# In each expert slot, y's squares and y's scaled copy move ahead of both halves of the next second weight's conversion

## The chip, the cores and the metric

The kernel runs on one core of one Trainium2 chip. The metric is the device time of one execution in microseconds (us), lower is better. In a program on one core that is the core's own time. The engines are named as in the profile: PE is TensorE, DVE is VectorE, ACT is ScalarE, POOL is GpSimd, SP is SyncE. ACTq and SPq stand for the queues from which ACT and SP issue transfers.

## What is computed

The reference is three layers in a row. The change touches only the second.

```python
# 1. attention with a state per head: for every step t (S = 768), B = 4, H = 8, D = 48
y[:, :, t] = einsum('bhd,bhde->bhe', q[:, :, t], state)
state = state + bt * einsum('bhd,bhe->bhde', kt, vt - einsum('bhde,bhd->bhe', state, kt))
# 2. mixture of 8 experts, one for each token: x [3072, 384], w1 [8, 384, 1024], w2 [8, 1024, 384]
expert_idx = argmax(logits, axis=1)
for e in range(E):
    h = maximum(x[mask] @ w1[e], 0.0)
    out[mask] = gate_w[mask, None] * (h @ w2[e])
# 3. dense: w_in [384, 2048], w_out [2048, 384]
h = maximum(x @ w_in, 0.0)
return h * h @ w_out
```

## The kernel before

The program has three stages, one for each layer, each with a stream of instructions for every engine; semaphores set all order between engines. The order within an engine is the order in which its function is written, and an instruction that waits holds back everything written behind it on that engine.

The second stage, `experts`, is a loop over NS = 31 slots. A slot is a tile of 128 tokens that all go to one expert. Its work, for slot j:

- PE: `up(j)` is x @ w1 in two halves of 24 matmul passes each (L1356). Then `turn_x(j + 1)` transposes the next tile's x (L1345). Then `down(j)` is h @ w2, 24 matmuls of 384 columns (L1367): each of the 8 blocks of h takes three, since h and w2 are both held as a high and a low part. `down(j)` waits for both parts of the first half of h (`s_ht[0]`), for the low part of the first half of w2 (`s_w2_lo`), and for the y of the slot before (`s_ys`). After 12 of its matmuls it waits again, for the second halves. `down` is followed by `up(j + 1)` with nothing between.
- ACT: `high_h(j, 0)` and `high_h(j, 1)` write the high part of h (L1406), each when PE's half of `up(j)` is done. `take_xt(j + 1)` copies the transposed x (L1393). Then come `high_w2(j + 1, 0)` and `high_w2(j + 1, 1)`, which convert the two halves of the next slot's second weight to its high part (L1402), and `square_y(j)` (L1422), which takes the sum of the squares of y. At the end ACT waits for the scaled y and issues its store (L1448).
- DVE: `low_h(j, 0)` and `low_h(j, 1)` write the low part of h (L1473). `low_w2(j + 1, 0)` and `low_w2(j + 1, 1)` subtract the high part of w2 from w2 (L1467), each when ACT's conversion is there. `keep_y(j)` makes a factor from the sum of the squares in two small steps (L1158, L1159) and writes the scaled copy of y (L1484).
- SP: for each slot a load of x, of w2 (L1022) and of w1 (L1018), 1536 KB each for the weights, into one of two buffers. Weights equal to those that the buffer holds aren't loaded again; such an issue is short.

The first half of w2's parts may be overwritten once 12 matmuls of `down(j)` are done (`s_y_half`), the second half once all 24 are (`s_y_ps`). The load of w2 for slot j + 2 goes into the buffer of slot j and waits for `low_w2(j, 1)`, which DVE does in the turn of slot j - 1; the load of w1 for slot j + 2 waits for `up(j)`.

In a few slots ACT and DVE have more to do ahead of the w2 conversion: tables and gates of the routing in slots 0 to 6 (an exponential in slot 3), squares of the dense weights in slots 10 to 15 and 20 to 25, and their conversion in slots 17 to 19 and 27 to 29. The dense weights' own loads are issued by POOL in slots 9 to 14 and 17 to 19.

Of the kernel before, what the change touches and what calls it, by code (L numbers as in the profile page):

```python
# [28 lines left out]
def wait(eng, sem, value):  # L29
    if count(value):  # L30
        eng.wait_ge(sem, value)
# [1123 lines left out]
def inverse_root(dve, step, out, shifted, squares, power):  # L1155

    magic = float(0x5f3759df + int(power * 2 ** 23))
    step(dve.tensor_scalar(shifted, squares.bitcast(I32), 1, None, ALU.arith_shift_right))  # L1158
    return dve.tensor_scalar(out.bitcast(I32), shifted, -1.0, magic, ALU.mult, ALU.add)  # L1159
# [18 lines left out]
def experts(nc, sh, cs, ctx, w1, w2, w_in, w_out, sorted_x, sorted_y, keep, rt, dense):  # L1178

    NT, NS, NS1, NS2, KD, DM, F1, F2, E, B = sh.NT, sh.NS, sh.NS1, sh.NS2, sh.KD, sh.DM, sh.F1, sh.F2, sh.E, sh.B  # L1180
# [82 lines left out]
    def piece_landed(n):  # L1263

        return 16 * sum(len(piece_parts(i)) for i in range(n % 2, n + 1, 2))

    def piece(n):
        return raw[:, n % WS * SW:(n % WS + 1) * SW]

    def part(n, which):  # L1270
        cols = slice(n % WS * SW, (n % WS + 1) * SW)
        if n < WS:
            return win[:, which].rearrange("p k f -> p (k f)")[:, cols]
        return wout[:, which].rearrange("p k d -> p (k d)")[:, cols]

    def squared(j):
        return j - SQUARE_IN if SQUARE_IN <= j < SQUARE_IN + WS else \
            j - SQUARE_OUT + WS if SQUARE_OUT <= j < SQUARE_OUT + WS else None

    def split(j):  # L1280
        for first, at in ((0, SPLIT_IN), (WS, SPLIT_OUT)):
            if at <= j < at + WS // 2:
                return [first + 2 * (j - at), first + 2 * (j - at) + 1]
        return []

    def scaled(j):
        return 0 if j == SQUARE_IN + WS else 1 if j == SQUARE_OUT + WS else None
# [3 lines left out]
    @block.sync  # L1291
    def _(sp):
        for j in range(1, NS):
            u = j % 2
            wait(sp, s_xt_ps, j - 1)
            if j == NS1:
                sp.wait_ge(rt.s_slots, 2)
                rt.scattered(sp, NT)
                sp.wait_ge(s_tails, 16 * E)
            rt.load_x(sp, sorted_x, j)  # L1300
            e = rt.expert(sp, j)
            fresh = rt.fresh(sp, j) if j > 1 else None
            wait(sp, s_w2_lo, 2 * j - 2)
            rt.load_w2(sp, w2, e, u, fresh)
            wait(sp, s_h_ps, 2 * j - 2)
            rt.load_w1(sp, w1, e, u, fresh)

        sp.wait_ge(s_store[0], 16 * ((NS + 1) // 2))
        sp.wait_ge(s_store[1], 16 * (NS // 2))
# [79 lines left out]
    @block.scalar  # L1389
    def _(act):  # L1390
        def take_xt(j):
            act.wait_ge(s_xt_ps, j + 1)
            act.copy(xs_t[:, :, :], ps[:, 0, 0:DM].rearrange("p (k t) -> p k t", k=KD)).then_inc(s_xt, 1)  # L1393

        def high_w2(j, half):
            if half == 0:
                act.wait_ge(s_w2[j % 2], 16 * (j // 2 + 1))
                wait(act, s_y_half, j)
            else:
                wait(act, s_y_ps, j)  # L1400
            ks = slice(half * HK, (half + 1) * HK)
            act.copy(w2_hl[:, 0, ks], w2_sb[j % 2][:, ks]).then_inc(s_w2_hi, 1)  # L1402

        def high_h(j, half):
            act.wait_ge(s_h_ps, 2 * j + half + 1)
            act.activation(ht_hl[:, 0, half * HK:(half + 1) * HK], ps[:, 1 + half, :].rearrange("p (k t) -> p k t", k=HK),  # L1406
                           ACT.Relu).then_inc(s_ht_hi, 1)

        def square_dense(n):
            act.wait_ge(s_raw[n % 2], piece_landed(n))  # L1410
            wait(act, s_dense_sq, n)
            act.activation(squares[:, :], piece(n), ACT.Square, accum_out=dense_ss[:, n:n + 1]).then_inc(s_dense_sq, 1)

        def high_dense(n):
            act.wait_ge(s_scale, n // WS + 1)
            act.activation(part(n, 0), piece(n), ACT.Copy, scale=dense.scale[:, n // WS:n // WS + 1])\
               .then_inc(s_dense_hi, 1)

        def square_y(j):
            act.wait_ge(s_y_ps, j + 1)  # L1420
            wait(act, s_y_ss, j)
            act.activation(y_squares[:, :], ps[:, 3, 0:DM], ACT.Square, accum_out=y_ss[:, j % 2:j % 2 + 1])\  # L1422
               .then_inc(s_y_ss, 1)

        take_xt(0)
        high_w2(0, 0)
        high_w2(0, 1)
        for j in range(NS):
            high_h(j, 0)
            high_h(j, 1)  # L1430
            if j + 1 < NS:
                take_xt(j + 1)
            if j == 1:
                act.activation(per_token[:, 0], ssx[:, :], ACT.Sqrt).then_inc(s_root, 1)
            if j == 3:
                act.wait_ge(s_exp, 1)
                act.activation(per_pair[:, 1], per_pair[:, 0], ACT.Exp).then_inc(s_exp, 1)
            if squared(j) is not None:
                square_dense(squared(j))
            for n in split(j):  # L1440
                high_dense(n)
            if j + 1 < NS:
                high_w2(j + 1, 0)
            square_y(j)
            if j + 1 < NS:
                high_w2(j + 1, 1)
            act.wait_ge(s_ys, j + 1)
            act.dma_start(sorted_y[j * P:(j + 1) * P, :], ys[:, j % 2]).then_inc(s_store[j % 2], 16)  # L1448

    @block.vector  # L1450
    def _(dve):
        done = [0]

        def step(ins):

            done[0] += 1
            ins.then_inc(s_step, 1)
            dve.wait_ge(s_step, done[0])
# [11 lines left out]
        def low_h(j, half):  # L1470
            dve.wait_ge(s_ht_hi, 2 * j + half + 1)
            ks = slice(half * HK, (half + 1) * HK)
            dve.scalar_tensor_tensor(out=ht_hl[:, 1, ks], in0=ps[:, 1 + half, :].rearrange("p (k t) -> p k t", k=HK),  # L1473
                                     scalar=0.0, in1=ht_hl[:, 0, ks].bitcast(F32), op0=ALU.max, op1=ALU.subtract)\
               .then_inc(s_ht[half], 1)

        def keep_y(j):
            dve.wait_ge(s_y_ss, j + 1)
            if j == 0:
                dve.wait_ge(s_pad, 1)  # L1480
            wait(dve, s_store[j % 2], 16 * (j // 2))
            factor = ys[:, j % 2, DM:DM + 1]
            step(inverse_root(dve, step, factor, shifted[:, 0:1], y_ss[:, j % 2:j % 2 + 1], dense.PART))
            dve.tensor_scalar(ys[:, j % 2, 0:DM], ps[:, 3, 0:DM], factor, None, ALU.mult).then_inc(s_ys, 1)  # L1484
# [13 lines left out]
        def low_dense(n):  # L1498
            dve.wait_ge(s_dense_hi, n + 1)
            dve.scalar_tensor_tensor(out=part(n, 1), in0=piece(n), scalar=dense.scale[:, n // WS:n // WS + 1],  # L1500
                                     in1=part(n, 0), op0=ALU.mult, op1=ALU.subtract).then_inc(s_dense_lo, 1)

        def ends():
            dve.wait_ge(rt.s_base, LAST + 2)
            step(dve.tensor_scalar(end_f[:, :], rt.base[:, :], cst[:, cs.LANE:cs.LANE + 1], None, ALU.add))
            dve.tensor_copy(end_row[:, :], end_f[:, :]).then_inc(s_ends, 1)
# [56 lines left out]
        def gates():  # L1563
            dve.wait_ge(s_exp, 2)
            step(dve.tensor_reduce(tok[8], per_pair[:, 1], AX.X, ALU.add))
            step(dve.tensor_scalar(tok[1], tok[8], 1e-9, None, ALU.add))
            step(dve.reciprocal(rt.gate[:, :], tok[1]))
# [28 lines left out]
        for j in range(NS):  # L1596
            low_h(j, 0)
            low_h(j, 1)
            if j == 0:
                for i in range(rt.RANK):  # L1600
                    rt.rank(dve, count_ps[:, 0:rt.CW], LAST, i)
                ends()
            if j == 1:
                late_rows()
            if j == 2:
                late_table()
            if j == 3:
                shift_logits()
            if j == 5:
                gates()  # L1610
            if j == 6:
                places_back()
            if scaled(j) is not None:
                scale_dense(scaled(j))
            for n in split(j):
                low_dense(n)
            if j + 1 < NS:
                low_w2(j + 1, 0)
            keep_y(j)
            if j + 1 < NS:  # L1620
                low_w2(j + 1, 1)


# [268 lines left out]
```

## Time and profile before

| | |
|---|---|
| median of 3 runs | 1139.73 us (1139.12 to 1146.21) |
| the profiled execution | 1139.16 us |
| its span, first to last instruction | 1137.4 us |
| PE busy | 1066.1 us (94%) |
| DVE busy | 673.9 us (59%) |
| ACT busy | 586.3 us (52%) |
| first `down` to last `down` of the experts stage | 429.55 to 732.29 us |

Times in the trace are counted from the start of the span; 1.76 us of the execution lie outside it. The experts stage takes its share from about 420 to 739 us. An engine's busy share over the whole span mixes three stages with different limits, so the stage has to be read by itself. A bracket at the end of a row of the timeline says how long the engine sat idle ahead of it and what ended that; no bracket means that it didn't wait. A group in which the first instruction waited says so for the first alone.

### The profile page before, as it was taken

The page shows a single profiled execution, that of the slowest core. Times are in us where ns is not written, and L with a number is a line of the kernel's source. Part 1 is how long each engine was busy: PE and PEld are TensorE (multiplying, and loading weights), DVE is VectorE, ACT ScalarE, POOL GpSimd, SP SyncE. Part 2 cuts the span into 40 slices and gives each one's busy share as a digit, 9 for nine tenths or more (in the row PEclk, how much of TensorE's full clock was granted, in tenths as well). Part 3 has the DMA queues.
Part 4 walks back from the last instruction along what each step waited for, and adds up shares of the span by engine and source line. Part 5 has one row for each costly group of instructions (what it writes and reads, how often), then busy time and mean ns, then how long its engine had stood idle before and what let it go on. Part 6 is the DMA issues. An engine that isn't in the chain of part 4 may idle for free. (4 is left out here: it accounts for less than half of the span.)

```text
span 1137.4 us, 25340 instructions
## 1 busy us (share of the span) xinstructions
PE 1066.1 (94%) x10332; PEld 828.4 (73%) x10332; DVE 673.9 (59%) x1381; ACT 586.3 (52%) x1229; POOL 322.8 (28%) x292
## 2 busy tenths in 40 slices
PE   3799999999999879999999999979999999999998
PEld 1577888888887779999999999835555555555554
DVE  5688888888888626665557556634443434343333
ACT  2577677777776644455656566523333333333332
POOL 5466767777766622200003000041010100000000
PEclk9899999999999969999999999979999999999999
DMA  7122123333231059999989871031010100000000
GB/s 115 22 43 46 35 39 71 86 79 70 67 85 51 9 194 397 391 388 392 394 293 376 293 261 37 23 93 30 29 29 2 49 8 29 1 29 1 28 1 28
DMA packets 130563, 131.19 MB, mean 115 GB/s; under 512 B 78280, under 2 KB 116880, under 8 KB 130448
## 3 DMA queue, kind: packets, MB, share of 16 engines
q1 hardware_dynamic: 120448, 105.72, 29.6%
q0 software_dynamic: 5536, 17.50, 4.5%
q10 hardware_dynamic: 4464, 6.35, 1.5%
q8 instruction: 82, 1.34, 0.5%
q14 instruction: 33, 0.27, 0.1%
HBM read 129.90 MB, written 21.68 MB: 133 GB/s over the span
## 5 line engine op out<-in xcount | busy, mean ns | idle before, releaser
L1736 PE MATMUL mlp_ps<-xg_t,win 128*128 128x512 f16 x864 | 201.8, 381 | 1.0 <-DVE xg_t L1816 1.0
L1747 PE MATMUL mlp_ps<-wout,sq_hl 128*128 128x384 f16 x1152 | 200.9, 326 | 0.0
L1356 PE MATMUL expert_ps<-xs_t,w_sb 128*128 128x128 f32 x1488 | 173.7, 277 | 4.7 <-issue 4.1
L1356 PEld LDWEIGHTS expert_ps<-xs_t,w_sb 128*128 128x128 f32 x1488 | 171.9, 194 | 7.1 <-issue 6.0
L1747 PEld LDWEIGHTS mlp_ps<-wout,sq_hl 128*128 128x128 f16 x1152 | 112.7, 98 | 83.4
L1736 PEld LDWEIGHTS mlp_ps<-xg_t,win 128*128 128x128 f16 x864 | 84.9, 98 | 93.7 <-issue 1.9
L1823 DVE TENSOR_TENSOR sq<-relu 128x512 f32<-128x512 f32 x96 | 66.5, 692 | 138.0 <-ACT relu L1773 136.7
L1467 DVE TENSOR_TENSOR w_hl<-w_sb,w_hl 128x1536 fp32r<-128x1536 f32 x62 | 108.6, 1753 | 54.4 <-ACT w_hl L1402 54.3
L1367 PE MATMUL expert_ps<-w_hl,ht_hl 128*128 128x384 f32 x744 | 137.4, 339 | 0.6 <-issue 0.6
L831 DVE TENSOR_TENSOR p_cur<-newt,cst 128x256 f16<-128x256 f32 x288 | 108.8, 419 | 46.6 <-PE newt L445 43.1
L1773 ACT ACTIVATE relu<-mlp_ps 128x512 f32<-128x512 f32 x96 | 57.3, 597 | 146.6 <-PE mlp_ps L1736 145.1
L1367 PEld LDWEIGHTS expert_ps<-w_hl,ht_hl 128*128 128x128 f32 x744 | 128.3, 188 | 0.8 <-issue 0.8
L655 ACT CAST t_cur<-newt 128x256 f16<-128x256 f32 x240 | 78.1, 375 | 69.0 <-PE newt L458 64.5
L1825 DVE TENSOR_TENSOR sq_hl<-sq,sq_hl 128x512 f16<-128x512 f32 x96 | 66.4, 692 | 65.6 <-ACT sq_hl L1779 62.9
L1402 ACT CAST w_hl<-w_sb 128x1536 fp32r<-128x1536 f32 x62 | 91.0, 1470 | 23.8 <-PE expert_ps L1367 22.3
L1779 ACT CAST sq_hl<-sq 128x512 f16<-128x512 f32 x96 | 59.3, 618 | 76.0 <-DVE sq L1823 76.0
L662 ACT CAST tt_cur<-newtt 128x512 f16<-128x512 f32 x144 | 86.2, 599 | 20.5 <-PE newtt L462 20.5
L1698 POOL DMA_INDIRECT gathered<-sorted_y,back x24 | 23.4, 974 | 258.0 <-PE mlp_ps L1710 133.2
L809 DVE SCALAR_TENSOR_TENSOR aq<-front_ps,beta_t,cst 128x256 f32<-128x256 f32 x192 | 83.7, 477 | 10.3 <-PE front_ps L431 10.0
L1406 ACT ACTIVATE ht_hl<-expert_ps 128x512 fp32r<-128x512 f32 x62 | 37.1, 598 | 93.4 <-PE expert_ps L1356 92.2
L462 PE MATMUL newtt<-tt_cur,p_cur 128*128 128x64 f16 x1152 | 73.9, 194 | 2.1 <-DVE p_cur L831 2.1
L431 PE MATMUL front_ps<-kq_t 48*128 48x256 f32 x384 | 71.6, 452 | 3.0 <-ACT kq_t L647 3.0
(222 smaller groups left out, 1638.4 us busy)
## 6 DMA issues: line engine op xcount, KB each, us to landing
w_sb<-in_moe_w SPq DMA_DIRECT2D x62, 1536.0 KB
sorted_y<-ys ACTq DMA_DIRECT2D x31, 200.0 KB
xs<-sorted_x SPq DMA_DIRECT2D x31, 192.0 KB
k_raw<-in_k SPq DMA_DIRECT2D x24, 192.0 KB, 3.0
q_pad<-in_q SPq DMA_DIRECT2D x24, 192.0 KB, 3.8
v_raw<-in_v SPq DMA_DIRECT2D x24, 192.0 KB, 4.0
out<-o_sb SPq DMA_DIRECT2D x6, 768.0 KB, 3.5
sorted_x<-zeros SPq DMA_DIRECT2D x11, 384.0 KB, 4.1
```

Source lines behind the costliest of these rows:

```text
L431: mm = pe.matmul(front_ps[:, i, 0:2 * P], kq_t[rows, n % B, p, 0:P], kq_t[rows, n % B, p, :], start=True, stop=True)
L462: mm = pe.matmul(newtt[:, h * HB:(h + 1) * HB], p_cur[:, level - 1, h], odd_blocks(tt_cur[:, n % 2, h:h + 1], level), start=True, stop=True)
L655: act.copy(even_blocks(t_cur[:, n % 2, HALF[hf]], level), blocks_of(newt[:, hf, 0:4 * HB], level))\
L662: act.copy(odd_blocks(tt_cur[:, n % 2], level), blocks_of(newtt[:, :], level)).then_inc(s_tt, 1)
L809: ins = dve.scalar_tensor_tensor(out=aq[:, n % B, h, :], in0=front_ps[:, i, 0:2 * P], scalar=beta_cols(n, slice(h, h + 1)).rearrange("p h ...
L831: dve.tensor_tensor(even_blocks(p_cur[:, level - 1, HALF[hf]], level), blocks_of(newt[:, hf, 0:4 * HB], level), kept.to_broadcast([P, 4] + ...
L1356: mm = pe.matmul(ps[:, 1 + half, c * P:(c + 1) * P], w1_sb[j % 2][:, kd, f], xs_t[:, kd], start=(kd == 0), stop=(kd == KD - 1))
L1367: mm = pe.matmul(ps[:, 3, 0:DM], ht_hl[:, a, k], w2_hl[:, b, k], start=(k == 0 and a + b == 0), stop=(k == K1 - 1 and a == 1))
L1402: act.copy(w2_hl[:, 0, ks], w2_sb[j % 2][:, ks]).then_inc(s_w2_hi, 1)
L1467: dve.tensor_tensor(w2_hl[:, 1, ks], w2_sb[j % 2][:, ks], w2_hl[:, 0, ks].bitcast(F32), ALU.subtract)\
L1736: mm = pe.matmul(ps[:, 4 + f % 2, :], win[:, a, kd, f * P:(f + 1) * P], xg_t[:, par, b, kd], start=(kd == 0 and a + b == 0), stop=(kd == K ...
L1747: mm = pe.matmul(ps[:, t, 0:DM], sq_hl[:, f % RING, a, t * P:(t + 1) * P], wout[:, b, f], start=(f == 0 and a + b == 0), stop=(f == K2 - 1 ...
```

## The change

In the loop over slots, `square_y(j)` on ACT now stands in front of `high_w2(j + 1, 0)` instead of between the two halves, and `keep_y(j)` on DVE in front of `low_w2(j + 1, 0)` in the same way. No instruction is added or removed, and every instruction keeps its waits.

```diff
@@ the loop over slots, on ScalarE
             for n in split(j):
                 high_dense(n)
+            square_y(j)
             if j + 1 < NS:
                 high_w2(j + 1, 0)
-            square_y(j)
-            if j + 1 < NS:
                 high_w2(j + 1, 1)
             act.wait_ge(s_ys, j + 1)
@@ the loop over slots, on VectorE
             for n in split(j):
                 low_dense(n)
+            keep_y(j)
             if j + 1 < NS:
                 low_w2(j + 1, 0)
-            keep_y(j)
-            if j + 1 < NS:
                 low_w2(j + 1, 1)
```

On ScalarE an ordinary slot reads as follows before the change (`w_hl` is `w2_hl`, `ht_hl` the parts of h):

```order
L1393 COPY xs_t<-expert_ps 128x384
L1402 CAST w_hl<-w_sb 128x1536
L1422 ACTIVATE y_squares,y_ss<-expert_ps 128x384
L1402 CAST w_hl<-w_sb 128x1536
L1448 DMA sorted_y<-ys 128x400
L1406 ACTIVATE ht_hl<-expert_ps 128x512 x2
```

and after it, with line numbers one lower from the moved line on:

```order
L1393 COPY xs_t<-expert_ps 128x384
L1422 ACTIVATE y_squares,y_ss<-expert_ps 128x384
L1402 CAST w_hl<-w_sb 128x1536 x2
L1447 DMA sorted_y<-ys 128x400
L1406 ACTIVATE ht_hl<-expert_ps 128x512 x2
```

The activation that reads the whole of y now stands ahead of both conversions. On VectorE an ordinary slot before the change:

```order
L1473 SCALAR_TENSOR_TENSOR ht_hl<-expert_ps,ht_hl 128x512 x2
L1467 TENSOR_TENSOR w_hl<-w_sb,w_hl 128x1536
L1158 TENSOR_SCALAR shifted<-y_ss 128x1
L1159 TENSOR_SCALAR ys<-shifted 128x1
L1484 TENSOR_SCALAR ys<-expert_ps,ys 128x384
L1467 TENSOR_TENSOR w_hl<-w_sb,w_hl 128x1536
```

and after it:

```order
L1472 SCALAR_TENSOR_TENSOR ht_hl<-expert_ps,ht_hl 128x512 x2
L1158 TENSOR_SCALAR shifted<-y_ss 128x1
L1159 TENSOR_SCALAR ys<-shifted 128x1
L1483 TENSOR_SCALAR ys<-expert_ps,ys 128x384
L1466 TENSOR_TENSOR w_hl<-w_sb,w_hl 128x1536 x2
```

The three steps on y stand ahead of both subtractions, which are now neighbours and lie directly ahead of the two steps on h.

## Rows read from the trace of the kernel before

**Rows 1.** Stretches: length; busy PE, PEld, DVE, ACT, POOL; clock; DMA share; GB/s
```profile
470.80:549.80 79.00, 78.95 (x599) 78.98 (x600) 47.62 (x70) 41.15 (x59) 5.44 (x8) 1.00 1.04 389
600.30:643.50 43.20, 40.00 (x302) 39.42 (x301) 29.60 (x34) 26.93 (x37) 10.62 (x20) 1.00 1.04 382
...
421.70:429.10 7.40, 7.38 (x48) 7.38 (x49) 4.13 (x4) 3.31 (x3) 0.52 (x2) 0.72 0.90 299
```

**Rows 2.** Timeline of PE: the ends of the stage, and slots 8 and 9
```profile
421.72 7.59 PE L1356 MATMUL expert_ps<-xs_t,w_sb 128*128 128x128 f32 x48 [0.57 <-ACT xs_t L1393]
429.55 4.41 PE L1367 MATMUL expert_ps<-w_hl,ht_hl 128*128 128x384 f32 x24
...
510.33 4.44 PE L1367 MATMUL expert_ps<-w_hl,ht_hl 128*128 128x384 f32 x24
514.61 5.52 PE L1356 MATMUL expert_ps<-xs_t,w_sb 128*128 128x128 f32 x48
520.21 4.44 PE L1367 MATMUL expert_ps<-w_hl,ht_hl 128*128 128x384 f32 x24
...
732.29 4.43 PE L1367 MATMUL expert_ps<-w_hl,ht_hl 128*128 128x384 f32 x24
```

**Rows 3.** Timeline of ACT in the same slot 8
```profile
512.78 1.48 ACT L1402 CAST w_hl<-w_sb 128x1536 fp32r<-128x1536 f32 x1 [1.53 <-PE expert_ps L1367]
514.80 0.49 ACT L1422 ACTIVATE y_squares<-expert_ps 128x384 f32<-128x384 f32 x1 [0.55 <-PE expert_ps L1367]
515.19 0.20 ACT L1422 ACTIVATION_READ_ACCUMULATOR y_squares<-expert_ps 128x1 f32 x1
515.28 1.46 ACT L1402 CAST w_hl<-w_sb 128x1536 fp32r<-128x1536 f32 x1
517.48 0.60 ACT L1406 ACTIVATE ht_hl<-expert_ps 128x512 fp32r<-128x512 f32 x1 [0.73 <-PE expert_ps L1356]
```

**Rows 4.** Timeline of DVE in slot 8
```profile
514.29 1.76 DVE L1467 TENSOR_TENSOR w_hl<-w_sb,w_hl 128x1536 fp32r<-128x1536 f32 x1 [2.68 <-ACT w_hl L1402]
515.96 0.15 DVE L1158 TENSOR_SCALAR shifted<-y_ss 128x1 int32<-128x1 int32 x1
...
516.87 1.75 DVE L1467 TENSOR_TENSOR w_hl<-w_sb,w_hl 128x1536 fp32r<-128x1536 f32 x1
518.53 0.68 DVE L1473 SCALAR_TENSOR_TENSOR ht_hl<-expert_ps,ht_hl 128x512 fp32r<-128x512 f32 x1
```

**Rows 5.** Timeline of all engines from slot 3 to slot 4
```profile
464.33 1.46 ACT L1402 CAST w_hl<-w_sb 128x1536 fp32r<-128x1536 f32 x1
465.82 1.76 DVE L1467 TENSOR_TENSOR w_hl<-w_sb,w_hl 128x1536 fp32r<-128x1536 f32 x1 [1.79 <-ACT w_hl L1402]
468.39 1.75 DVE L1467 TENSOR_TENSOR w_hl<-w_sb,w_hl 128x1536 fp32r<-128x1536 f32 x1
470.06 1.28 DVE L1473 SCALAR_TENSOR_TENSOR ht_hl<-expert_ps,ht_hl 128x512 fp32r<-128x512 f32 x2
470.85 4.40 PE L1367 MATMUL expert_ps<-w_hl,ht_hl 128*128 128x384 f32 x24 [0.59 <-issue]
475.29 0.49 ACT L1422 ACTIVATE y_squares<-expert_ps 128x384 f32<-128x384 f32 x1 [0.55 <-PE expert_ps L1367]
```

**Rows 6.** Timeline of DVE: both halves back to back, before slot 0
```profile
423.07 3.42 DVE L1467 TENSOR_TENSOR w_hl<-w_sb,w_hl 128x1536 fp32r<-128x1536 f32 x2 [1.36 <-ACT w_hl L1402]
```

**Rows 7.** Timeline of SP and PE: weight loads, and the slots that wait for them
```profile
518.90 0.37 SPq L1022 DMA_DIRECT2D w_sb<-in_moe_w  x1
...
590.50 4.42 PE L1367 MATMUL expert_ps<-w_hl,ht_hl 128*128 128x384 f32 x24
...
599.05 0.37 SPq L1022 DMA_DIRECT2D w_sb<-in_moe_w  x1
...
637.86 5.60 PE L1356 MATMUL expert_ps<-xs_t,w_sb 128*128 128x128 f32 x48 [1.51 <-issue]
643.53 4.43 PE L1367 MATMUL expert_ps<-w_hl,ht_hl 128*128 128x384 f32 x24
```

## Prediction

> **What bounds the kernel now.** I read the stage of the experts alone, since the change touches no other. The first view is busy time by stretches. From 470.80 to 549.80 us PE is busy for 78.95 of 79.00 us, while VectorE (DVE) has 47.62 us of work and ScalarE (ACT) 41.15 [rows 1]. So PE sets the pace, and the two others matter only through the moment at which they deliver. The DMA engines are also full there (share 1.04, 389 GB/s), which makes them a second candidate. The second view is the timeline of one ordinary slot, from the first matmul of `down(8)` at 510.33 to that of `down(9)` at 520.21: a period of 9.88 us [rows 2]. All periods below are taken between such starts. From the first `down` to the last, 429.55 to 732.29, there are 30 periods in 302.74 us [rows 2].
>
> The third view is what stands beside PE in that slot. Today ACT starts the first conversion at 512.78, when only half of `down` is done, squares y at 514.80 as soon as `down` is finished, and converts the second half from 515.28 [rows 3]. DVE subtracts at 514.29 and 516.87, with the steps on y from 515.96 in between, and does the low part of h at 518.53 for 0.68 us [rows 4]. That is the last thing `down(9)` needs, and it is there at 519.21. PE arrives at 520.21. The margin is 1.00 us. The question is whether the change eats it.
>
> **What the change moves.** No work is added. The square needs all of `down(j)`, and ACT works in order, so the first conversion can no longer start at half of `down(j)`; it queues behind the square. That costs it 515.28 - 512.78 = 2.50 us [rows 3]. On DVE the y steps leave the place between the two subtractions, which shortens that part: 516.87 - 515.96 = 0.91 us [rows 4]. The delay wins by 1.59 us, and the margin is 1.00, so `down` has to wait some 0.6 us. For the sum I want it closer.
>
> The new chain, link by link, from one `down` to the next:
>
> 1. First matmul of `down` to the start of the square: 475.29 - 470.85 = 4.44 us [rows 5]. I take this pair and not 510.33 to 514.80 (4.47) [rows 2, 3], because here `down` had started after a wait, as it will in the new kernel.
> 2. Square to the conversion behind it: 515.28 - 514.80 = 0.48 [rows 3].
> 3. Conversion to the first subtraction, when DVE is already waiting: 465.82 - 464.33 = 1.49 [rows 5].
> 4. First subtraction to the second, back to back: the pair takes 3.42 and one takes 1.75, so 1.67 [rows 4, 6].
> 5. Second subtraction to the low part of h: 470.06 - 468.39 = 1.67 [rows 5].
> 6. Low part of h to PE's start, when PE is already waiting: 470.85 - 470.06 = 0.79 [rows 5].
>
> The sum is 10.54 us, against 9.88. PE would stand still about 0.66 us per slot ahead of `down`. Three things could be later than this chain, and aren't. The y steps start when the square's accumulator has been read, 515.19 + 0.20, and take 0.91, so they end 1.50 us after the square's start; the subtraction comes 1.97 after it (links 2 and 3). The second conversion ends at most 0.48 + 2 x 1.46 = 3.40 after the square's start; the second subtraction comes at 1.97 + 1.67 = 3.64. The high part of h on ACT was ready to go at 517.48, which is 2.68 after the square; now ACT is free for it at about 3.40, plus the issue of the store, which I put at no more than 0.50; with its 0.60 it ends by 4.50, and DVE wants it at 5.31 (links 2 to 5) [rows 3, 4].
>
> Link 4 is where I weigh the notes. The row shows that the second subtraction starts 0.08 us before the end of the first (1.67 against 1.75). The Trainium skill, "VectorE: DVE Perf Modes", section "The DRAIN you can't avoid", says that the next operation doesn't start until the pipeline is empty. By that rule links 4 and 5 would be 0.08 longer each and the total some 4.8 us higher; this trace doesn't agree with so strict a reading, and I keep the row.
>
> 30 periods of 10.54 are 316.2 us, against 302.74: **+13.5 us**. This takes in the slots that already had a longer period, since the chain replaces their period instead of adding to it. The extra work on ACT and DVE in some slots (dense weights, routing) stands ahead of the square and ends before `down` does, so it hides as now. After the last slot nothing changes.
>
> **The weight loads.** SP waits for the second subtraction before it issues the w2 load, and w1's load is queued behind that on SP. Now the subtraction ends at 516.87 + 1.75 = 518.62 and the load goes out at 518.90 [rows 4, 7], 8.57 us after the slot's `down`. In the new order it ends 4.44 + 0.48 + 1.49 + 1.67 + 1.75 = 9.83 after `down`, so the load goes out at 10.11, about 1.55 later. In most slots that is harmless: weights are asked for more than a slot ahead, and PE has 0.66 us more per slot. Late in the stage it isn't. From 600.30 to 643.50 the DMA share is 1.04 at 382 GB/s while PE is busy only 40.00 of 43.20 us [rows 1]; POOL's loads of the dense weights come on top, and `up(21)` waits 1.51 us, until 637.86 [rows 7]. The run of full transfers begins with the load at 599.05, in slot 16, whose `down` starts at 590.50. From there `up(21)` is 47.36 us away and `down(21)` 53.03. If the whole queue starts 1.55 later, `down(21)` comes at 54.58, where five chains of 10.54 need 52.70: **+1.9 us**. Bounds: 0, if the queue catches up, and 3.5, if the dense loads, which wait for DVE, bring a second delay of the same size.
>
> Total: 13.5 + 1.9 = +15.4 us. The profiled execution took 1139.16 us, so 1154.6; on the median of 1139.73 it is 1155.1. I say 1155.0.
>
> **The rivals.**
>
> *The loads set the pace, so PE's wait is free.* The DMA share of 1.04 from 470.80 to 549.80 speaks for it. Then only the slots from `down(21)` at 643.53 on would pay: 9 x 10.54 - (732.29 - 643.53) = +6.1 us, 1145.8 us, within 1%. It decides if the loads alone need 10.54 us per slot. Against it: PE stood idle for 0.05 us in those 79 [rows 1], so a weight load ended no wait there. Chance 0.07.
>
> *VectorE's shorter stretch is worth more than the late start.* This is the case on the other side. Between slots 3 and 4 the conversion was late anyway, and from its start at 464.33 to `down` at 470.85 it took 6.52 us; links 3 to 6 make 5.62 [rows 5]. So there the 0.91 us off DVE is a true saving. It decides in every slot whose first conversion starts less than 0.91 us ahead of where the square lets it. In the ordinary slot it starts 2.50 ahead [rows 3]. If the square were let go so early that the delay vanished, most slots would stay at 9.88 and the time at 1139; if all 30 gained the whole 0.91 us as well, it would be 27 us less, 1112. Chance 0.05, of which 0.02 for more than 1% faster.
>
> *The late loads hurt in every full stretch.* If each load's 1.55 us came through in a few more slots, say four, 6 us more: 1161. Against it: PE's own slower pace. Chance 0.05.
>
> *The clock falls.* At 421.70 to 429.10, after a pause, PE was granted 0.72 of full speed, between the levels of 1.2 and 2.4 GHz, and one `up` took 7.59 us instead of 5.52 [rows 1, 2]. With 2.07 us in each of 30 slots the time would be 1217 us. The stretch with the wait of 1.51 us kept 1.00, the upper level [rows 1, 7], and the new waits are shorter, so 0.01. The Trainium skill, "TensorE: Matmul & The Clock Gate", section "HAM oscillation — how this bites in real kernels", describes kernels that fall back to half speed through pauses in TensorE's work, again and again; the pauses of this trace didn't do it.
>
> **How the numbers follow.** The forecast itself has 0.82. An error of 0.02 in each of five links makes 0.1 x 30 = 3 us either way. With the loads' bounds that is 13.5 - 3 + 0 = +10.5 to 13.5 + 3 + 3.5 = +20, or 1150 to 1160. The two nearer rivals lie outside, with less than 0.2 together. What a measurement of this kernel can tell from no change is about 1%, 11.4 us, so the line is at 1151.1. Slower by over 1%: 0.82 + 0.05 + 0.01, less 0.02 for the forecast's lower end, 0.86. Within 1%: 0.07 + 0.03 + 0.02, 0.12. Faster: 0.02.
>
> **What the new profile would show.** PE idle 0.6 to 0.7 us ahead of L1367 in nearly every slot, with periods of 10.54 us. The two conversions back to back behind the square, ACT idle 2 us longer ahead of it. DVE's two subtractions back to back, followed by the low part of h without a wait. `down(21)` at about 429.55 + 224 us, with waits on w1 only near it. If `down` starts without a wait, links 1 to 6 overlap where I put them in a row; if PE waits ahead of `up` in many slots, it is the loads.

## The result, and the profile after

The changed kernel took a median of 1159.92 us in 4 runs (1158.48 to 1161.88), against 1142.90 us for the kernel before, also in 4 runs: a ratio of 1.0155, with a 95% interval of 1.0127 to 1.0183. A second set of 4 runs gave 1161.81 us beside 1141.93, a ratio of 1.0177 (1.0142 to 1.0212). So the change costs 17 to 20 us, where +15.4 was forecast. The direction was as forecast; the size was above it. The first median lies at the upper end of the range that was given (1150 to 1160, with 1155.0 as the forecast), and the second is above that range.

The profiled execution took 1160.28 us, 21.1 us more than that of before. First the timeline of all engines around slot 8 of the changed kernel, which answers to [rows 2 to 4] (rows in between are left out at the dots):

```profile
513.43 4.43 PE L1367 MATMUL expert_ps<-w_hl,ht_hl 128*128 128x384 f32 x24 [0.46 <-issue]
...
517.70 5.52 PE L1356 MATMUL expert_ps<-xs_t,w_sb 128*128 128x128 f32 x48
517.89 0.49 ACT L1422 ACTIVATE y_squares<-expert_ps 128x384 f32<-128x384 f32 x1 [4.24 <-PE expert_ps L1367]
...
518.37 1.46 ACT L1402 CAST w_hl<-w_sb 128x1536 fp32r<-128x1536 f32 x1
518.51 0.15 DVE L1158 TENSOR_SCALAR shifted<-y_ss 128x1 int32<-128x1 int32 x1 [4.50 <-ACT y_squares L1422]
...
519.87 3.43 DVE L1466 TENSOR_TENSOR w_hl<-w_sb,w_hl 128x1536 fp32r<-128x1536 f32 x2 [0.36 <-ACT w_hl L1402]
521.11 0.60 ACT L1406 ACTIVATE ht_hl<-expert_ps 128x512 fp32r<-128x512 f32 x1
...
523.21 1.36 DVE L1472 SCALAR_TENSOR_TENSOR ht_hl<-expert_ps,ht_hl 128x512 fp32r<-128x512 f32 x2
...
523.58 0.37 SPq L1022 DMA_DIRECT2D w_sb<-in_moe_w  x1
...
524.00 4.42 PE L1367 MATMUL expert_ps<-w_hl,ht_hl 128*128 128x384 f32 x24 [0.46 <-issue]
```

Read it downwards. ACT waits 4.24 us for the end of `down(8)`, squares, and converts. DVE does its y steps, waits 0.36 us for the first conversion, subtracts twice without a gap, and goes straight to the low part of h at 523.21. PE starts `down(9)` 0.79 us after that. The period is 524.00 - 513.43 = 10.57 us, against 9.88 before. Nothing in the chain has slack, which is why the brackets of DVE and PE are short: a busy chain shows up as many small waits on the engine at its end, here 0.46 us in each slot. The period grew by more than that bracket, 0.69 us, because the recorded end of the transpose (L1345) reached 0.24 us into `down` in the kernel before and no longer does.

Second, the timeline of PE from slot 12 to slot 13. This has no counterpart in the kernel before, where `up(13)` followed `down(12)` with no wait of note:

```profile
555.70 4.40 PE L1367 MATMUL expert_ps<-w_hl,ht_hl 128*128 128x384 f32 x24 [0.16 <-issue]
563.48 8.48 PE L1356 MATMUL expert_ps<-xs_t,w_sb 128*128 128x128 f32 x48 [3.37 <-issue]
...
572.04 4.42 PE L1367 MATMUL expert_ps<-w_hl,ht_hl 128*128 128x384 f32 x24
```

`up(13)` waited 3.37 us and then ran for 8.48 us instead of 5.52. The period is 16.34 us. The same two numbers by stretches (columns as in [rows 1]):

```profile
556.00:566.00 10.00, 6.63 (x36) 6.34 (x35) 4.92 (x6) 4.58 (x7) 0.04 (x1) 0.84 1.03 388
566.00:576.00 10.00, 10.00 (x64) 10.00 (x64) 1.38 (x2) 2.61 (x5) 0.53 (x1) 0.82 1.01 359
576.00:586.00 10.00, 9.54 (x74) 9.34 (x73) 5.63 (x7) 5.83 (x9) 0.00 (x0) 1.00 0.72 250
```

PE was without work, and then its granted clock was 0.84 and 0.82 on average, a mix of 1.00 (2.4 GHz) and half of it (1.2 GHz). The DMA engines were full until `up(13)` began, which points to a load as what PE waited for: `up(13)` reads w1, and w1's load stands behind w2's on SP. The experiment e4_split_after tests this.

Third, PE in slots 20 and 21, which answers to [rows 7]:

```profile
641.12 5.60 PE L1356 MATMUL expert_ps<-xs_t,w_sb 128*128 128x128 f32 x48 [1.28 <-issue]
...
652.96 5.60 PE L1356 MATMUL expert_ps<-xs_t,w_sb 128*128 128x128 f32 x48 [1.73 <-issue]
...
658.64 4.42 PE L1367 MATMUL expert_ps<-w_hl,ht_hl 128*128 128x384 f32 x24
```

From first to last `down` the 30 periods now take 324.73 us (428.97 to 753.70) against 302.74. They divide cleanly: 27 of them are 10.54 to 10.58, with a mean of 10.56. Thirty such make +14.1 us. The period of slot 12 is 5.8 above the mean. Those of slots 19 and 20 (11.36 and 11.85) are 2.1 above twice the mean together. The sum is 22.0. The first stage took 0.6 us less in this execution than in that of before. PE's waits for loads in slots 20 and 21, 1.28 and 1.73 us, are no longer than in the kernel before, whose trace has 1.69 us ahead of `up(20)` beside the 1.51 ahead of `up(21)` [rows 7].

### The profile page after: what moved, and what is told of

The parts are those of the page before. It is cut to its first block and busy times, and to the rows that moved or that the text cites. A ratio compares the mean times of both kernels' runs of the same rounds, so it can differ in the third digit from the quotient of the medians.

```text
span 1158.5 us, 25338 instructions
## 1 busy us (share of the span) xinstructions
PE 1073.4 (93%) x10332; PEld 831.8 (72%) x10332; DVE 676.8 (58%) x1381; ACT 581.2 (50%) x1229; POOL 322.6 (28%) x292
## 3 DMA queue, kind: packets, MB, share of 16 engines
q8 instruction: 82, 1.34, 0.5%
## 5 line engine op out<-in xcount | busy, mean ns | idle before, releaser
L1356 PE MATMUL expert_ps<-xs_t,w_sb 128*128 128x128 f32 x1488 | 177.2, 281 | 7.1 <-issue 6.4
L1356 PEld LDWEIGHTS expert_ps<-xs_t,w_sb 128*128 128x128 f32 x1488 | 175.8, 197 | 9.0 <-issue 8.0
L1466 DVE TENSOR_TENSOR w_hl<-w_sb,w_hl 128x1536 fp32r<-128x1536 f32 x62 | 106.2, 1755 | 12.1 <-ACT w_hl L1402 12.1
L1402 ACT CAST w_hl<-w_sb 128x1536 fp32r<-128x1536 f32 x62 | 87.9, 1468 | 0.0
L458 PE MATMUL newt<-p_cur,tt_cur 128*128 128x64 f16 x960 | 63.7, 195 | 9.1 <-DVE p_cur L831 8.8
```

The source lines that it names most:

```text
L1356: mm = pe.matmul(ps[:, 1 + half, c * P:(c + 1) * P], w1_sb[j % 2][:, kd, f], xs_t[:, kd], start=(kd == 0), stop=(kd == KD - 1))
L1466: dve.tensor_tensor(w2_hl[:, 1, ks], w2_sb[j % 2][:, ks], w2_hl[:, 0, ks].bitcast(F32), ALU.subtract)\
```

## The experiments

Each kernel was timed beside the kernel before on the same chip. Two causes had to be told apart and sized: the chain through the square and the subtractions, and the loads that go out later.

**Only ScalarE's half of the change (e1_act_only).** `square_y(j)` moves, `keep_y(j)` stays.

```diff
 on ScalarE
+            square_y(j)
             if j + 1 < NS:
                 high_w2(j + 1, 0)
-            square_y(j)
-            if j + 1 < NS:
                 high_w2(j + 1, 1)
```

> Only ScalarE's part of the change: the square ahead of both conversions, while VectorE keeps its steps on y between the two subtractions. Theory (one chain from down's end through the square, both subtractions and the low part of h sets the period): the 0.91 us of y steps come back into the chain, 10.54 + 0.91 = 11.45 us per slot, 30 x 11.45 - 302.7 = +41 us, about 1180 us, PE idle about 1.4 us ahead of L1367. Rival (the loads' delay makes most of the loss, the chain little): the loads go out 0.9 us later than in the changed kernel and the time is about as there, 1160 to 1165 us.

Measured: 1180.71 us, ratio 1.0359 (1.0335 to 1.0382). The timeline of PE:

```profile
509.10 4.43 PE L1367 MATMUL expert_ps<-w_hl,ht_hl 128*128 128x384 f32 x24 [1.36 <-issue]
513.37 5.52 PE L1356 MATMUL expert_ps<-xs_t,w_sb 128*128 128x128 f32 x48
...
520.58 4.40 PE L1367 MATMUL expert_ps<-w_hl,ht_hl 128*128 128x384 f32 x24 [1.36 <-issue]
```

The period is 11.48 us here and the 30 together take 343.81, +41.1 us. PE waits 1.12 to 1.43 us ahead of every `down` but the first, mostly 1.36, and never waits for a load. The chain alone makes this result to within 1 us, and the rival is out. The loads go out later in the slot than in the changed kernel, 11.06 us after `down` (SP at 520.16) against 10.15, and still cost nothing: at 11.46 us per slot they have the time. So in these runs a late load costs only where the pace leaves the transfers too little room.

**Only VectorE's half (e2_dve_only).** `keep_y(j)` moves, `square_y(j)` stays between the conversions.

```diff
 on VectorE
+            keep_y(j)
             if j + 1 < NS:
                 low_w2(j + 1, 0)
-            keep_y(j)
-            if j + 1 < NS:
                 low_w2(j + 1, 1)
```

> Only VectorE's part: the steps on y ahead of both subtractions, while ScalarE squares between its conversions as before. Theory (chain): the first subtraction starts about 1.53 us after the square instead of before it, the period is 4.45 + 1.53 + 1.67 + 1.67 + 0.79 = 10.1 us against 9.88, some +4 us over the slots that don't wait for loads, and the w2 load goes out 1.1 us later; 1143 to 1150 us, the upper end if the loads stall PE in slot 13 as in the changed kernel. Rival (the square on ScalarE is all the cost): no change from before, 1140 us.

Measured: 1146.63 us, ratio 1.0054 (1.0037 to 1.0071). Timeline of DVE:

```profile
516.67 0.15 DVE L1158 TENSOR_SCALAR shifted<-y_ss 128x1 int32<-128x1 int32 x1 [4.02 <-ACT y_squares L1422]
516.86 0.15 DVE L1159 TENSOR_SCALAR ys<-shifted 128x1 int32<-128x1 int32 x1
517.05 0.62 DVE L1484 TENSOR_SCALAR ys<-expert_ps,ys 128x384 f32<-128x384 f32 x1
517.58 3.42 DVE L1467 TENSOR_TENSOR w_hl<-w_sb,w_hl 128x1536 fp32r<-128x1536 f32 x2
520.92 0.69 DVE L1473 SCALAR_TENSOR_TENSOR ht_hl<-expert_ps,ht_hl 128x512 fp32r<-128x512 f32 x1
```

DVE now idles 4.02 us for the square, although the first conversion ended 1.16 us before DVE starts (ACT, 514.03 + 1.48). Most periods are 10.08 to 10.18, as the chain says. PE also waited for loads, 0.59 us ahead of `up(12)`, 1.34 ahead of `up(15)` and 1.94 ahead of `up(20)`. So neither half of the change is free: VectorE's half costs about 6 us by itself (its load waits included), yet gives back 0.9 us a slot when ScalarE's half is there.

**The old order with late loads (e3_loads_late).** SP asks for both conditions ahead of both loads.

```diff
 on SP
             wait(sp, s_w2_lo, 2 * j - 2)
-            rt.load_w2(sp, w2, e, u, fresh)
             wait(sp, s_h_ps, 2 * j - 2)
+            rt.load_w2(sp, w2, e, u, fresh)
             rt.load_w1(sp, w1, e, u, fresh)
```

> The order of before on every engine but SP: the w2 load also waits until up of the slot two ahead of it is done, so it goes out about 1.25 us later and w1 about 0.5 us later. The chain through ScalarE and VectorE is as before. Theory (late loads let the transfer queue run dry once in a slot, which costs bandwidth that slots 9 to 14 and 17 to 21 need): dips in GB/s once in a slot, waits of several us ahead of up in slots 13 to 15, 1145 to 1152 us. Rival (the wait in slot 13 of the changed kernel is chance, or comes from the slower pace): dips or not, the waits stay as before, 1140 to 1142 us.

Measured: 1145.46 us, ratio 1.0053 (1.0031 to 1.0074). The DMA engines' busy share and rate from 490 to 514 us in 40 slices of 0.6 us, of this kernel:

```profile
DMA  9999999999999999999889999999999999997999
GB/s 391 430 416 387 364 369 381 376 374 384 381 397 409 416 403 382 423 363 404 282 286 356 379 392 397 384 403 394 411 416 416 396 405 380 366 181 191 299 313 381
```

and of the kernel before, in the same window:

```profile
DMA  9999999999999999999999999999999999989999
GB/s 416 410 384 405 400 392 379 374 371 371 400 385 410 398 423 416 385 373 371 342 372 379 389 384 384 378 411 386 416 416 416 382 388 408 292 271 387 374 397 384
```

SP issued w2's load at 519.81, which is 10.12 us after the `down` at 509.69: 1.55 us later than before, more than the 1.25 expected, and the same as in the changed kernel (523.58 - 513.43 = 10.15). There is a dip in each slot, to 282 and 181 GB/s, where the kernel before has one to 342 and one to 271. PE waited 1.03 us ahead of `up(11)`, and 0.76, 2.03 and 1.78 ahead of `up(19)` to `up(21)`. The chain was untouched, so loads that go out 1.55 us later cost time by themselves: some 6 us by the ratio (its interval says 3.5 to 8.4), 3.1 us by the 30 periods of the one trace (305.88). The total fell at the lower end of what was expected, but not in the place: ahead of `up(13)` to `up(15)`, where waits of several us were expected, there are 0.22 us at most. So this run shows that late loads cost something, and doesn't reproduce the wait of the changed kernel in slot 13. The changed kernel shows such dips too, once in its 10.57 us, here from 500 to 520 us in slices of 0.5:

```profile
DMA  9799999969999999999999999971988999999999
GB/s 344 287 401 401 396 373 360 274 201 267 332 372 378 372 378 399 421 418 398 418 393 407 400 426 382 375 272 71 118 147 255 341 391 435 391 399 394 394 384 417
```

The mean rates don't show a loss of bandwidth. From 450 to 540 us, first of the kernel before, then of the changed one (columns as in [rows 1]):

```profile
450.00:540.00 90.00, 88.88 (x675) 88.30 (x673) 58.28 (x97) 46.85 (x68) 9.34 (x11) 1.00 1.04 391
450.00:540.00 90.00, 86.25 (x635) 84.64 (x636) 54.55 (x93) 42.23 (x64) 9.34 (x11) 1.00 1.00 365
```

The same bytes per slot at the slower pace make 391 x 9.88 / 10.56 = 366 GB/s, so the lower rate is what the chain's pace alone gives. The kernel of this experiment, at the old pace, moved 387.

**The changed kernel with w2's load in two halves (e4_split_after).** The first half's load needs only the first subtraction.

```diff
 on SP, with load_w2 and its count of landings adapted
-            wait(sp, s_w2_lo, 2 * j - 2)
-            rt.load_w2(sp, w2, e, u, fresh)
+            for half in range(2):
+                wait(sp, s_w2_lo, 2 * j - 3 + half)
+                rt.load_w2(sp, w2, e, u, fresh, half)
```

> The changed kernel with each w2 load cut into two halves, the first of which waits for the first subtraction alone, so that it goes out about 8.4 us after down's start (as in the kernel before, 8.57) instead of 10.15. Theory (late loads): no wait of 3.4 us ahead of up(13) and no half clock behind it (5.8 us less), less waiting in slots 19 to 21 (up to 2 us less); what stays is the chain, 30 x 10.56: 1152 to 1155 us. Rival (the wait in slot 13 comes from something else): 1160 us, as the changed kernel.

Measured: 1155.81 us, ratio 1.0138 (1.0116 to 1.0160). The 30 periods take 319.32 us. No wait for a load is left up to slot 19, and `up(13)` follows at once:

```profile
554.95 4.42 PE L1371 MATMUL expert_ps<-w_hl,ht_hl 128*128 128x384 f32 x24 [0.46 <-issue]
559.22 5.52 PE L1360 MATMUL expert_ps<-xs_t,w_sb 128*128 128x128 f32 x48
...
565.52 4.42 PE L1371 MATMUL expert_ps<-w_hl,ht_hl 128*128 128x384 f32 x24 [0.46 <-issue]
```

That agrees with late loads as the cause in slot 13. Only the first half of w2 goes out early, 8.48 us after `down` (521.17 - 512.69); w1's load goes out 10.60 us after it (512.72 - 502.12), as in the changed kernel (10.62) and later than before (9.83), and yet PE finds w1 in time. The interval of the ratio overlaps with that of the changed kernel, but the slowest of the 4 executions (1156.98) is below the fastest of the changed kernel's 8 (1158.48). The second part of the expectation fell: `up(20)` and `up(21)` still waited 1.50 and 1.79 us. Those waits have another cause. Nor are the dips gone: from 500 to 520 us this kernel's rate falls to 166 and 117 GB/s in slices of half a microsecond. So a dip by itself doesn't make PE wait.

**The changed kernel again (e5_after_again).**

> The changed kernel once more, for a second trace. If the wait of 3.4 us ahead of up(13) and the half clock behind it belong to the schedule (late loads in slots 9 to 14), this trace shows them again, in slot 12, 13 or 14, and the time is near 1160 us. If they were chance, the trace has no such wait and its time lies near 1155 us.

Measured: 1161.81 us, ratio 1.0177 (1.0142 to 1.0212). Timeline of PE:

```profile
562.02 4.43 PE L1367 MATMUL expert_ps<-w_hl,ht_hl 128*128 128x384 f32 x24 [0.46 <-issue]
567.57 5.60 PE L1356 MATMUL expert_ps<-xs_t,w_sb 128*128 128x128 f32 x48 [1.13 <-issue]
573.00 0.49 PE L1345 MATMUL expert_ps<-cst,xs 128*128 128x128 f32 x3
573.25 4.42 PE L1367 MATMUL expert_ps<-w_hl,ht_hl 128*128 128x384 f32 x24
```

The wait stands in the same slot in both traces, which speaks for the schedule as its cause. Its size isn't set by the schedule alone: it is 1.13 us here, and `up(13)` ran for 5.60 us, without the slowdown of the first trace, so the period is 11.23 instead of 16.34. The 30 periods take 319.80 us, +17.1. This execution still took 1162.29 us, because its first `down` began at 435.29 and not at 428.97: the first stage was 6.3 us longer. The change doesn't touch the first stage, so such a shift isn't laid to it.

**The low part of h between the subtractions (e6_hfirst).** The changed kernel, with VectorE's last link shortened.

```diff
 on VectorE, in the changed kernel; low_h(0, 0) is done once ahead
                 low_w2(j + 1, 0)
+                low_h(j + 1, 0)
                 low_w2(j + 1, 1)
 and at the top of the next turn
-            low_h(j, 0)
             low_h(j, 1)
```

> The changed kernel with one more exchange on VectorE: the low part of the first half of h stands between the two w2 subtractions instead of behind both, so down(j + 1) needs one subtraction less before it starts. Theory (chain): low part of h ends about 9.0 us after down's start, before PE arrives; period 9.88 us, no idle time ahead of L1367, and 14 us come back. The second subtraction then ends at 10.7 us and the w2 load goes out at about 10.9, later than in any kernel so far, at the full pace: waits ahead of up in slots 10 to 15 and 19 to 21, so 1146 to 1153 us in all. Rival (PE's wait comes from ScalarE's lateness and not from VectorE's row of steps): period stays 10.56, 1160 us.

Measured: 1148.93 us in 10 runs, ratio 1.0051 (1.0035 to 1.0067). Timeline of PE, `down(8)` and `down(9)`:

```profile
511.38 4.44 PE L1367 MATMUL expert_ps<-w_hl,ht_hl 128*128 128x384 f32 x24
...
521.26 4.44 PE L1367 MATMUL expert_ps<-w_hl,ht_hl 128*128 128x384 f32 x24
```

Periods without a load wait are 9.88 us again, with no wait ahead of `down`, so it was VectorE's row of steps that held PE. The loads go out later still, 10.97 us after `down` (SP at 522.35), and PE waits for them ahead of `up` in slots 1, 3, 6, 12, 15 and 19 to 21, 0.38 to 2.26 us each; the 30 periods take 313.45.

**The same, with w2's load in halves (e7_hfirst_split).**

> The kernel of e6_hfirst with each w2 load cut into halves, the first going out about 8.4 us after down's start. Theory (chain and late loads are the two costs, and each has its cure): period 9.88, few extra waits for loads, 1140 to 1146 us, that is 14 to 19 us below the changed kernel and close to the kernel before. Rival (late loads matter only where the second half is late too): as e6_hfirst, 1146 to 1153 us.

Measured: 1142.83 us in 10 runs, ratio 1.0000 (0.9982 to 1.0019). The interval is clear of that of e6_hfirst, so here the halves alone give back some 6 us: the firmest sign that late loads cost time. Each cost has its cure, and together they bring the changed order back to the time of the kernel before. The 30 periods take 303.70 us. They still hold a wait of 2.42 us ahead of `up(20)`.

**The kernel before, with w2's load in halves (e8_split_before).**

> The kernel before with each w2 load cut into halves, the first going out about 2.6 us earlier. The transfer queue never runs dry in slots 2 to 16 there, so an earlier load adds no bandwidth: 1139 to 1142 us, no change. If the kernel before also lost time to late loads, 2 to 4 us less.

Measured: 1141.04 us in 10 runs, ratio 0.9989 (0.9967 to 1.0012), no change, as expected. The waits moved: 0.77 us ahead of `up(15)` and 2.74 ahead of `up(21)`.

**The second dense weight's loads spread (e9_spread_after).** What makes PE wait in slots 19 to 21? POOL issues two dense pieces in each of slots 17 to 19, beside a full pair of expert weights.

```diff
 on GpSimd, in the kernel with the changed order and halved loads
                 pool.wait_ge(s_dense_lo, n - WS + 1)
+                pool.wait_ge(s_h_ps, 2 * (SPLIT_IN + 1 + n - WS))
```

> The kernel of e4_split_after (changed order, w2 loads in halves) with the six loads of the second dense weight spread: one for each slot from 17 to 22 instead of two for each of 17 to 19. Theory (the waits of 1.5 and 1.8 us ahead of up(20) and up(21) come from two dense pieces beside a full pair of expert weights): those waits shrink by 2 us or more in sum, periods of 10.56 to 10.8 us in slots 19 to 21, 1153 to 1154 us. Rival (they come from the late start of the expert loads): no change from e4_split_after.

Measured: 1152.67 us, ratio 1.0095 (1.0079 to 1.0110). Timeline of PE in slots 20 and 21:

```profile
636.14 5.52 PE L1361 MATMUL expert_ps<-xs_t,w_sb 128*128 128x128 f32 x48
...
642.45 4.42 PE L1372 MATMUL expert_ps<-w_hl,ht_hl 128*128 128x384 f32 x24 [0.46 <-issue]
646.71 5.52 PE L1361 MATMUL expert_ps<-xs_t,w_sb 128*128 128x128 f32 x48
```

All 30 periods lie between 10.54 and 10.58 us, 316.90 in sum, and PE waits for no load from `up(1)` on. This is the change's chain alone: 316.90 - 302.74 = +14.2 us in the stage. The medians of this experiment differ by less, 10.8 us (1152.67 against 1141.91); the 302.74 is from a single trace of the kernel before, which has load waits of its own.

**The same edit in the order of before (e10_spread_before).**

> The kernel of e8_split_before (order of before, w2 loads in halves) with the loads of the second dense weight spread as in e9_spread_after. Theory: the 2 to 3 us that PE waits ahead of up(20) and up(21) go, 1136 to 1139 us beside a kernel before of 1140 to 1142, a version that beats both. Rival: the wait only moves to a later slot, no change.

Measured: 1137.54 us in 6 runs, ratio 0.9959 (0.9942 to 0.9975). The 30 periods take 298.01 us, and one wait for a load is left, 0.62 us ahead of `up(15)`. It is 0.4% below the kernel before, clear of the noise, and below the changed one. Against it the changed order with the same loads (1152.67) is 15.1 us slower by the medians and 18.9 us by the 30 periods. That is the price of the chain where no load wait hides a part of it. The spread loads weren't tried without the halves.

## Why the prediction was right or wrong

**The chain was right.** The new periods were forecast link by link, and the six links were to make 10.54 us; 27 of the 30 periods measure 10.54 to 10.58. The same links gave 11.45 for ScalarE's half alone (measured: 343.81 / 30 = 11.46) and 10.1 for VectorE's half (most 10.08 to 10.18). The term was put at +13.5 us and measured +14.1, and +14.2 with all load waits taken away. The 0.02 us by which each slot exceeds the sum was within the error that the prediction gave a link. The sign to look for, PE idle for 0.6 to 0.7 us ahead of `down`, shows in the period (+0.68) and not in the bracket (0.46).

**The margin was read rightly.** `down` waited for the low part of h: with that step one place earlier the period fell from 10.56 to 9.88.

**The weight loads were the step that failed.** The prediction said that the later load "in most slots" is "harmless", since weights are asked for more than a slot ahead and PE has 0.66 us more per slot, and put its cost at nothing up to slot 16. The load did go out as late as forecast (10.15 us after `down`, forecast 10.11), and up to `up(12)` it was harmless: no wait for a load. In slots 9 to 14, where the same DMA engines move the dense pieces as well, it wasn't, and PE waited ahead of `up(13)`. That term was missing: 5.8 us in the first trace (3.37 us of waiting, and 3.0 of a slower `up` behind it, less what the chain would have made PE wait anyway), 0.7 in the second. The prediction compared when a load goes out with when it must land, and left out the other transfers in between. An obvious suspect is a queue that runs nearly dry: in the changed kernel the rate falls to 71 GB/s in one slice of half a microsecond between 500 and 520 us, where the kernel before falls to 254. But e4_split_after has deep dips as well and doesn't wait ahead of `up(13)`, so how a later issue turns into a late load in slot 13 stays open. Shown is that the wait went when w2's load was halved, that the late loads alone, in the old order, cost 0.5%, and that halving gave back 0.5% in the order of e6_hfirst.

The term for slots 19 to 21 had the right size for the wrong reason, which is luck. It was +1.9, and the two traces show 2.1 and 2.3. The prediction laid it to the 1.55 us by which the first load of that stretch starts later. Halved loads removed that lateness for the first half of w2, though not for w1, and the waits stayed (1.50 and 1.79 us). Spreading the dense loads, on top of the halves, removed them. They come from two dense pieces beside each pair of expert weights, and the kernel before has waits of that size too.

**The rivals.** That the loads set the pace and PE's wait is free is refuted: with every load wait gone, the chain still costs 14.2 us in the stage, and 10.8 by the medians. That VectorE's shorter stretch outweighs the delay is refuted too, though it is real: without VectorE's half the chain is 0.9 us per slot longer. "The late loads hurt in every full stretch" (1161 us, given 0.05) was the nearest to the measured time, and it deserved more; but by its reason it was only partly right, since the loads hurt in one slot beyond those of the forecast and not in four. The falling clock was given 0.01, as something that would happen in every slot. In the changed kernel it happened once, in one of two traces, behind the wait of 3.37 us, and cost 8.48 - 5.52 = 3.0 us; behind the waits of 0.46 us it never did. That is the kind of fall that the Trainium skill, "TensorE: Matmul & The Clock Gate", section "HAM oscillation — how this bites in real kernels", describes for pauses in TensorE's work, and here the first trace of the changed kernel agrees with it, in one slot.

**The rule on consecutive VectorE operations** that was set aside would have put the total 4.8 us higher by links 4 and 5. The pair of subtractions took 3.43 us in the changed kernel, with single ones of 1.75, and the low part of h starts 3.34 us after the first: the row decides, and the new trace has the same overlap of 0.08 us. That this rule's total, 1155.0 + 4.8, comes out near the measured time is chance: its periods would be 10.70 us, and they are 10.56.

**Open.** Why the same schedule makes PE wait 3.37 us in one execution and 1.13 in another wasn't settled. Nor was it shown at what wait the clock falls: in other kernels here `up` took 7.22 or 7.23 us behind waits of 1.94, 2.19, 2.26 and 2.42 us, and 5.59 or 5.60 behind waits of 1.98, 2.03, 2.16 and 2.74. The trace of e2_dve_only has a mean granted clock of 0.81 from 630 to 639 us, around such an `up`. The term of the loads rests on two traces of the changed kernel, and the 302.74 us of the kernel before on one.

## What to carry to other kernels

When an operation is moved ahead of another on an in-order engine, compute the whole chain up to the engine that sets the pace and compare it with the margin there: here a start 2.50 us later minus 0.91 us of shorter work, against 1.00 us. Then follow the moved completion to whatever waits for it to free a buffer: where the transfers have little room, a later issue can cost time even when no single load seems late. Look for it in the stretches in which a second stream of transfers uses the same DMA engines, and not in the mean rate, which falls with the pace. Here a load cut in two, so that its first half needs only the first half of its buffer, gave 4 to 6 us back, and spreading the transfers of the second stream over more slots took away the waits that were left.

## What the runs showed of the hardware that wasn't expected

- The DMA engines kept a busy share of 1.00 from 450 to 540 us while they moved 365 GB/s, against 1.04 and 391 GB/s in the kernel before. The drop is what the longer slots give with the same bytes (366 GB/s), so a share of 1.00 doesn't tell that the engines move as much as they can.
- One wait can cost twice. The 3.37 us ahead of `up(13)` were followed by an `up` of 8.48 us, at a granted clock of 0.82 to 0.84 in the mean of the two stretches around it.
- The first `down` of the experts stage, ahead of which the kernels do the same but for a halved first load, began between 428.17 and 435.29 us into the span in the twelve traces of this study. So single executions can differ by 0.6% before the changed part begins. The sum of the 30 periods leaves that out, though it isn't exact either: the changed kernel's two traces have 324.73 and 319.80.
